# Splitting the wait of the score block and ordering its matmuls by head parity in a linear-attention and two-layer MoE kernel

## The chip, the cores and the metric

The kernel runs on one core of a Trainium2 chip. A core has five engines that run side by side, each through its own instructions in order: PE (TensorE, matrix multiplies), DVE (VectorE), ACT (ScalarE), POOL (GpSimd) and SP (SyncE, which here only issues DMA transfers). They order each other through semaphores. The metric is the device time of one execution in microseconds, lower is better.

## The reference, cut to what matters

Three layers follow each other: a recurrent attention over 768 steps for 4 x 8 (batch, head) pairs with a head dimension of 48, and two mixture-of-experts layers over the 3072 tokens. The change touches the first alone.

```python
B, H, S, D = r.shape                       # 4, 8, 768, 48
state = np.zeros((B, H, D, D))
for t in range(S):
    kt, vt, rt, wt = k[:, :, t], v[:, :, t], r[:, :, t], w[:, :, t]
    cur = np.einsum('bhd,bhe->bhde', u[None] * kt, vt)
    y[:, :, t] = np.einsum('bhd,bhde->bhe', rt, state + cur)
    state = wt[:, :, :, None] * state + np.einsum('bhd,bhe->bhde', kt, vt)
# then: top-1 MoE with softmax gate (8 experts, 384 -> 1024 -> 384),
# then: capacity-bound assignment by sorted logits and a second MoE of the same size
```

## The kernel before

**Tiling.** The attention works on 24 chunks of 128 time steps (`NT`): six chunks (`C`) for each of four batch elements, all eight heads together. Heads go in pairs: `PR = 4` pairs `a`, and in a pair head `g = 0` lies on partitions 0 to 63 and head `g = 1` on partitions 64 to 127 (48 dimensions padded to `HP = 64`). With cumulated decays a chunk becomes a masked product of keys and receptances (the scores), times values, plus the carried state.

**One chunk, over the engines.** DVE scans the decays (`scan_after`, `scan_before`), makes `k_dec` (`decay_k`, line 682, signals `s_kdec`), `rk`, and masks the scores (`mask_scores`, line 698). POOL makes `r_dec` (line 467, `s_rdec`). PE computes the scores in `score` (lines 814 to 825): for each pair and each `g` one float32 matmul of the 64 rows of `k_dec` and `r_dec` of that half, with 128 columns, into PSUM tile `p_g[0]` or `p_g[1]`. The last matmul of either tile signals `s_g`. DVE's `mask_scores(t)` waits for `s_g` twice, once for a tile, writes `scores` and signals `s_masked` twice. `values(t)` on PE multiplies the masked scores with the values.

**Order of the work.** The orders are written by hand, one loop over `t` for each engine. PE's loop in step `t` runs `score(t+1)`, `diag_sums(t+1)`, `update(t)` (state), `x_forward(t-1)`, `diag_back(t+1)`, `values(t)`, `logits(t-1)`, now and then `counts`, `k_transposes(t+1)` (in each sixth chunk `scored`, a product of expert weights with the gate, in its place) and `x_back(t)`. DVE's loop in step `t` runs `take_x(t-1)`, both scans of `t+2`, `mask_scores(t+1)`, `add_state(t)`, `decay_k(t+2)`, `product(t+2)` and parts of the routing. ACT moves results out of PSUM between PE's blocks: `diag_evac` (line 539) between `diag_sums` and `diag_back`, `k_evac`, `carry` of the state, `check` of the decays. SP loads decays, keys and receptances three chunks ahead, values one.

**What guards the tiles.** `score(t)` waits for `s_kdec` and `s_rdec` of `t`, and before it overwrites `p_g` for both masks of chunk `t - 1`: `s_masked >= 2 * t`. `decay_k(t + 1)` waits for both `s_g` of `t - 1`, since it overwrites a `k_dec` buffer. Behind the last chunk `first_h` uses the two `p_g` tiles for the first rows of the expert layer.

Of the kernel before, what the change touches and what calls it, by code (L numbers as in the profile page):

```python
# [19 lines left out]
PR = H // 2  # L20
HP = 64
# [174 lines left out]
def attention(nc, general, sb, ps, sem, io, keep):  # L196
# [78 lines left out]
    s_g = sem("s_g")  # L275
    s_masked = sem("s_masked")
# [54 lines left out]
    with nc.Block() as block:  # L331
# [481 lines left out]
        def _(pe):  # L813
            def score(t):
                pe.wait_ge(s_kdec, t + 1)
                pe.wait_ge(s_rdec, t + 1)
                if t > 0:
                    pe.wait_ge(s_masked, 2 * t)
                for a in range(PR):
                    for g in range(2):  # L820
                        half = slice(HP * g, HP * g + HP)
                        ins = pe.matmul(p_g[g][:, a, :], k_dec[half, t % 2, a, :], r_dec[half, t % 3, a, :],
                                        start=True, stop=True)
                        if a == PR - 1:
                            ins.then_inc(s_g, 1)

            def x_forward(t):
                pe.wait_ge(s_x, t + 1)
# [141 lines left out]
            for t in range(-1, NT):  # L970
                if t + 1 < NT:
                    score(t + 1)
                    diag_sums(t + 1)
# [8 lines left out]
                if t == 1:  # L982
                    pe.wait_ge(s_norm, 10)
                    for a in range(KD):
                        ins = pe.transpose(p_e[:, a, :], emb[:, a * P:(a + 1) * P], ident[0:E, 0:E])
# [1505 lines left out]
```

## Time and profile before

| | us |
|---|---|
| median of 3 runs | 824.91 |
| lowest, highest | 824.82, 826.84 |
| the profiled execution | 824.82 |
| its span in the profile | 823.0 |
| PE busy | 779.0 (95%) |
| DVE busy | 437.2 (53%) |
| ACT busy | 322.5 (39%) |
| attention stage, about | 0 to 188 |

The profile shows one execution. For each engine it has the busy time, and for each idle stretch the event that ended it. A float32 matmul leaves two records of PE and two of its weight loads (PEld, which run beside PE's matmuls), a transpose one. The end of a matmul record is modelled: records overlap, so the time from one start to the next tells what a matmul costs in a stream, not its duration.

### The profile page before, as it was taken

What the parts mean: (1) busy time and instruction counts of PE and PEld (TensorE: products, weight loads), DVE (VectorE), ACT (ScalarE), POOL (GpSimd) and SP (SyncE); (2) the same over time, 40 slices, a digit from 0 to 9 for tenths busy, and PEclk for the clock granted to TensorE, in tenths of its full rate; (3) what the DMA queues carried; (4) which work ended last, traced back from release to release, by engine and by line L of the source; (5) the groups of instructions that cost most, each with busy time, mean ns of one, the idle gap of its engine ahead of it and who ended that gap; (6) DMA issues with size and microseconds to landing.
All of it is one profiled execution on the core that took longest, in us unless ns stands there. A gap on an engine that the chain in (4) does not pass through costs nothing. (4 is left out here: it accounts for less than half of the span.)

```text
span 823.0 us, 17288 instructions
## 1 busy us (share of the span) xinstructions
PE 779.0 (95%) x6003; PEld 563.0 (68%) x6004; DVE 437.2 (53%) x1194; ACT 322.5 (39%) x818; POOL 145.0 (18%) x151
## 2 busy tenths in 40 slices
PE   8999999997999999999999965999999999999996
PEld 7778787865777778887777744755565555555653
DVE  8889898934333233333332348475767667573000
ACT  4878787843344444444444420112121211112120
POOL 4124343430000000000000000103223140502201
PEclk9999999999999999999999985999999999999999
DMA  8889899525677565667575511341505052346100
GB/s 278 312 274 355 310 348 326 216 82 188 219 251 250 198 208 201 208 227 268 179 262 191 169 52 63 121 154 58 192 20 192 33 189 94 124 151 218 49 10 31
DMA packets 68850, 149.63 MB, mean 182 GB/s; under 512 B 4968, under 2 KB 37104, under 8 KB 68784
## 3 DMA queue, kind: packets, MB, share of 16 engines
q1 hardware_dynamic: 53952, 114.03, 39.4%
q0 software_dynamic: 6912, 23.75, 8.5%
q10 hardware_dynamic: 7920, 10.99, 4.1%
q8 instruction: 39, 0.64, 0.3%
q14 instruction: 27, 0.22, 0.1%
HBM read 130.06 MB, written 18.69 MB: 181 GB/s over the span
## 5 line engine op out<-in xcount | busy, mean ns | idle before, releaser
L1498 PE MATMUL p_o<-w2s,hid_t 128*128 (+1 forms) x432 | 152.1, 495 | 0.0
L1487 PEld LDWEIGHTS p_h<-x_t,w1s 128*128 128x128 f32 x1248 | 143.4, 192 | 7.2
L1487 PE MATMUL p_h<-x_t,w1s 128*128 128x128 f32 x1248 | 143.5, 275 | 0.0
L1971 PE MATMUL p_gh<-g_t,w1s 128*128 128x384 f32 x384 | 132.8, 494 | 0.0
L1987 PE MATMUL p_go<-w2s,g_hid 128*128 128x384 f32 x384 | 131.5, 489 | 0.0
L1498 PEld LDWEIGHTS p_o<-w2s,hid_t 128*128 128x128 f32 x432 | 78.7, 192 | 45.9 <-issue 0.9
L1971 PEld LDWEIGHTS p_gh<-g_t,w1s 128*128 128x128 f32 x384 | 70.0, 190 | 45.7 <-issue 6.1
L1987 PEld LDWEIGHTS p_go<-w2s,g_hid 128*128 128x128 f32 x384 | 70.3, 190 | 42.1
L1371 ACT ACTIVATE hid_t<-p_h 128x512 f32<-128x512 f32 x52 | 31.0, 597 | 155.2 <-PE p_h L1487 144.8
L1710 ACT ACTIVATE g_hid<-p_gh 128x384 f32<-128x384 f32 x64 | 31.4, 490 | 112.8 <-PE p_gh L1971 112.8
L1671 POOL DMA_INDIRECT g_in<-y_rows,table x24 | 29.6, 1232 | 252.2 <-DVE table L1830 247.3
L1424 DVE TENSOR_SCALAR col<-col 128x1 f32<-128x1 f32 x27 | 4.2, 154 | 130.5 <-ACT ex L1375 130.4
L1760 DVE TENSOR_TENSOR reach<-free_best,cand 128x3968 bf16<-128x3968 f32 (+2 forms) x19 | 58.6, 3083 | 0.6
L1681 POOL DMA_INDIRECT out<-o_row,table x24 | 40.1, 1672 | 79.6 <-ACT o_row L1703 44.8
L518 ACT ACTIVATE diag_v<-v_pad,diag 128x48 f32<-128x48 f32 x192 | 48.0, 327 | 0.0
L467 POOL TENSOR_TENSOR r_dec<-kr_t,decays 128x512 f32<-128x512 f32 x24 | 28.7, 1197 | 103.7 <-issue 60.4
L1703 ACT ACTIVATE o_row<-p_go 128x384 f32<-128x384 f32 x24 | 11.8, 490 | 87.7 <-PE p_go L1987 87.7
L1696 ACT ACTIVATE g_t<-p_gx 128x384 f32<-128x384 f32 x22 | 10.8, 490 | 75.4 <-PE p_gx L1958 75.4
L1375 ACT ACT_TABLE_LOAD x27 | 34.6, 1283 | 3.7 <-issue 3.2
L1822 DVE TENSOR_TENSOR row_is<-row_b,iota_p 128x2048 bf16<-128x2048 bf16 (+1 forms) x16 | 34.9, 2221 | 0.3
L1358 ACT ACT_TABLE_LOAD x27 | 34.6, 1283 | 0.5
L1331 POOL COPY w2s<-w2g 128x64 f32<-128x64 f32 x6 | 1.4, 236 | 185.2 <-PE p_o L1498 185.2
(269 smaller groups left out, 1052.7 us busy)
## 6 DMA issues: line engine op xcount, KB each, us to landing
w1s<-in_w SPq DMA_DIRECT2D x28, 1536.0 KB, 6.6
kr_t<-in_kr_t SPq DMA_DIRECT2D x24, 512.0 KB, 4.0
w2t<-in_w_t SPq DMA_DIRECT2D x16, 768.0 KB
w1s<-in_w1b SPq DMA_DIRECT2D x8, 1536.0 KB, 6.6
w2s<-in_w2b SPq DMA_DIRECT2D x8, 1536.0 KB
w2s<-in_w POOLq DMA_DIRECT2D x12, 768.0 KB, 6.5
w_pad<-in_w_t SPq DMA_DIRECT2D x24, 256.0 KB, 5.0
v_pad<-in_v_pad SPq DMA_DIRECT2D x24, 256.0 KB, 7.9
```

The source lines that it names most:

```text
L518: ins = act.activation(diag_v[:, t % 2, h, :], v_pad[:, q, h, 0:D], ACT.Copy, scale=diag[:, t % 2, h:h + 1])
L1358: act.activation(col[:, q, 0:1], col[:, q, 15:16], ACT.Sqrt).then_inc(s_root, 1)
L1371: act.activation(hid_t[:, half * g:half * (g + 1), :], p_h[g][:, :, :], ACT.Relu).then_inc(s_relu, 1)
L1375: act.activation(ex[:, :], lg[:, q, :], ACT.Exp, bias=col[:, q, 9:10], accum_out=col[:, q, 10:11]).then_inc(s_exp, 1)
L1487: ins = pe.matmul(p_h[g][:, m, :], w1s[:, q, a, f:f + P], x_t[:, q, a, :], start=(a == 0), stop=(a == KD - 1))
L1498: ins = pe.matmul(p_o[:, :], hid_t[:, m, :], w2s[:, bass.ds(half, 1), m, :].rearrange("p o n -> p (o n)"), start=(m == 0), stop=(m == KF - 1))
L1681: pool.indirect_dma_start(out=io["out"][:, :], out_offset=place(1, p, i), in_=o_row[:, p % 2, i, :], in_offset=None).then_inc(s_out[p % 2] ...
L1710: act.activation(hid[:, m, :], p_h[(KF * p + m) % 3][:, :], ACT.Relu).then_inc(s_relu, 1)
L1760: dve.tensor_tensor(reach(n)[:, at, :], free(p)[:, at].unsqueeze(2).broadcast_to([P, len(part), n]), cand[:, 0:n].unsqueeze(1).broadcast_t ...
L1822: dve.tensor_tensor(row_is[:, at, :], row_b[:, 1, at].unsqueeze(2).broadcast_to([P, size, P]), iota_p[:, :].unsqueeze(1).broadcast_to([P, ...
L1971: ins = pe.matmul(p_h[n % 3][:, :], w1s[:, p % 2, a, m * P:(m + 1) * P], x_t[:, a, :], start=(a == 0), stop=(a == KD - 1))
L1987: ins = pe.matmul(p_o[n % 2][:, :], hid[:, m, i * P:(i + 1) * P], w2s[:, p % 2, m, 0:HD], start=(m == 0), stop=(m == KF - 1))
```

## The change

In `score` the two loops change places: first the four matmuls of `g = 0`, then the four of `g = 1`. The wait on `s_masked` is split: ahead of the `g = 0` matmuls for the first mask of chunk `t - 1`, ahead of the `g = 1` matmuls for the second. `s_g` is signalled by the fourth and by the eighth matmul, where it was the seventh and the eighth. The matmuls themselves, their operands and their number stay.

```diff
             def score(t):
                 pe.wait_ge(s_kdec, t + 1)
                 pe.wait_ge(s_rdec, t + 1)
-                if t > 0:
-                    pe.wait_ge(s_masked, 2 * t)
-                for a in range(PR):
-                    for g in range(2):
-                        half = slice(HP * g, HP * g + HP)
+                for g in range(2):
+                    half = slice(HP * g, HP * g + HP)
+                    if t > 0:
+                        pe.wait_ge(s_masked, 2 * (t - 1) + g + 1)
+                    for a in range(PR):
                         ins = pe.matmul(p_g[g][:, a, :], k_dec[half, t % 2, a, :], r_dec[half, t % 3, a, :],
                                         start=True, stop=True)
-                        if a == PR - 1:
-                            ins.then_inc(s_g, 1)
+                    ins.then_inc(s_g, 1)
```

What stands in PE's order at a score block of the running loop, before. The row's end names the semaphores that the first matmul waits for; the block begins behind `x_back` (line 927) and ends at `diag_sums` (line 856):

```order
L927 MATMUL p_x<-ident,y_tr 128x128 [waits s_xTev,s_yev]
L927 MATMUL p_x<-ident,y_tr 128x128 x3
L822 MATMUL p_g0<-r_dec,k_dec 128x128 [waits s_masked,s_rdec,s_kdec]
L822 MATMUL p_g1<-r_dec,k_dec 128x128
L822 MATMUL p_g0<-r_dec,k_dec 128x128
L822 MATMUL p_g1<-r_dec,k_dec 128x128
L822 MATMUL p_g0<-r_dec,k_dec 128x128
L822 MATMUL p_g1<-r_dec,k_dec 128x128
L822 MATMUL p_g0<-r_dec,k_dec 128x128
L822 MATMUL p_g1<-r_dec,k_dec 128x128
L856 MATMUL p_diag<-rk,u_blk 32x128 [waits s_diag,s_rk]
```

And with the change, at the same place (line numbers behind the function are one lower):

```order
L926 MATMUL p_x<-ident,y_tr 128x128 [waits s_xTev,s_yev]
L926 MATMUL p_x<-ident,y_tr 128x128 x3
L822 MATMUL p_g0<-r_dec,k_dec 128x128 [waits s_masked,s_rdec,s_kdec]
L822 MATMUL p_g0<-r_dec,k_dec 128x128 x3
L822 MATMUL p_g1<-r_dec,k_dec 128x128 [waits s_masked]
L822 MATMUL p_g1<-r_dec,k_dec 128x128 x3
L855 MATMUL p_diag<-rk,u_blk 32x128 [waits s_diag,s_rk]
L855 MATMUL p_diag<-rk,u_blk 32x128 x3
```

The tiles `p_g0` and `p_g1` alternated; now four of one stand ahead of four of the other, with a wait between.

The first score block of the kernel, behind the filler matmuls of line 122, which has no wait on masks, before:

```order
L122 MATMUL p_y<-ones 128x128 x19
L822 MATMUL p_g0<-r_dec,k_dec 128x128 [waits s_kdec,s_rdec,s_shape,s_in]
L822 MATMUL p_g1<-r_dec,k_dec 128x128
L822 MATMUL p_g0<-r_dec,k_dec 128x128
L822 MATMUL p_g1<-r_dec,k_dec 128x128
L822 MATMUL p_g0<-r_dec,k_dec 128x128
L822 MATMUL p_g1<-r_dec,k_dec 128x128
L822 MATMUL p_g0<-r_dec,k_dec 128x128
L822 MATMUL p_g1<-r_dec,k_dec 128x128
L856 MATMUL p_diag<-rk,u_blk 32x128 [waits s_rk]
```

and with the change:

```order
L122 MATMUL p_y<-ones 128x128 x19
L822 MATMUL p_g0<-r_dec,k_dec 128x128 [waits s_kdec,s_rdec,s_shape,s_in]
L822 MATMUL p_g0<-r_dec,k_dec 128x128 x3
L822 MATMUL p_g1<-r_dec,k_dec 128x128 x4
L855 MATMUL p_diag<-rk,u_blk 32x128 [waits s_rk]
L855 MATMUL p_diag<-rk,u_blk 32x128 x3
```

Here too only the order within the block moved.

## Rows read from the trace of the kernel before

**Rows 1.** The page: busy tenths in 40 slices, and the granted clock

```profile
PE   8999999997999999999999965999999999999996
...
DVE  8889898934333233333332348475767667573000
...
PEclk9999999999999999999999985999999999999999
```

**Rows 2.** Table by stretch: from:to, length, busy of each engine; six chunks each

```profile
49.00:90.20 41.20, 40.54 (x551) 31.83 (x550) 37.69 (x75) 32.75 (x114) 14.46 (x11) 1.00 0.91 328
...
131.50:172.80 41.30, 40.59 (x551) 31.85 (x550) 34.16 (x71) 32.74 (x114) 14.85 (x12) 1.00 0.62 216
```

**Rows 3.** Timeline of PE, one chunk: start, length, line, tiles, count

```profile
108.17 0.63 PE L919 MATMUL p_kb<-ident,k_dec 128*128 128x128 f32 x4
108.64 0.60 PE L927 MATMUL p_x<-ident,y_tr 128*128 128x128 f32 x4
109.17 1.16 PE L822 MATMUL p_g<-r_dec,k_dec 64*128 64x128 f32 x16
110.27 0.43 PE L856 MATMUL p_diag<-rk,u_blk 128*32 128x128 f32 x8
...
116.02 1.16 PE L822 MATMUL p_g<-r_dec,k_dec 64*128 64x128 f32 x16
```

**Rows 4.** Waits of PE's weight loads, 8 to 176: total, times, longest

```profile
PEld p_diag L862 <- ACT diag_t L539: 4.4, 10, 1.8
PEld p_u L889 <- issue: 4.0, 20, 0.2
PEld p_y L847 <- issue: 3.9, 23, 0.2
...
PEld p_g L822 <- DVE k_dec L682: 2.9, 6, 0.8
```

**Rows 5.** Waits of PE's matmuls in the same stretch

```profile
PE p_g L822 <- DVE k_dec L682: 1.7, 3, 0.6
PE p_diag L862 <- ACT diag_t L539: 1.6, 1, 1.6
PE p_x L830 <- DVE rows L717: 0.3, 1, 0.3
```

**Rows 6.** Waits of DVE in the same stretch

```profile
DVE rows L717 <- PE p_x L927: 8.2, 4, 4.1
...
DVE scores L698 <- PE p_g L822: 0.3, 1, 0.3
```

**Rows 7.** Timeline of DVE over the same chunk

```profile
110.05 0.56 DVE L717 TENSOR_TENSOR rows<-p_x,diag_v 128x384 f32<-128x384 f32 x1
...
113.31 1.26 DVE L698 TENSOR_TENSOR scores<-p_g,mask 128x512 f32<-128x512 f32 x2
...
114.75 0.68 DVE L682 TENSOR_TENSOR k_dec<-kr_t,decays 128x512 f32<-128x512 f32 x1
```

**Rows 8.** Timeline of PE, one score block in growing cuts

```profile
102.79 0.38 PE L822 MATMUL p_g<-r_dec,k_dec 64*128 64x128 f32 x2 [0.59 <-DVE k_dec L682]
102.79 0.60 PE L822 MATMUL p_g<-r_dec,k_dec 64*128 64x128 f32 x6 [0.59 <-DVE k_dec L682]
102.79 1.16 PE L822 MATMUL p_g<-r_dec,k_dec 64*128 64x128 f32 x16 [0.59 <-DVE k_dec L682]
```

**Rows 9.** The score line's matmul (least, median, most), then full-height ones

```profile
L822 PE MATMUL p_g<-r_dec,k_dec x384: 272/272/373, 8.8 to 164.6; 64*128 64x128 f32 x192
...
184.03 2.75 PEld L965 LDWEIGHTS p_g<-x_t,w1s 128*128 128x128 f32 x24
184.05 2.92 PE L965 MATMUL p_g<-x_t,w1s 128*128 128x128 f32 x24
```

**Rows 10.** Timeline at the end of the stage

```profile
176.98 0.64 PE L927 MATMUL p_x<-ident,y_tr 128*128 128x128 f32 x4
...
187.00 0.96 POOL L478 DMA_INDIRECT sorted_rows<-rows,pos  x1 [2.47 <-DVE pos L770]
```

## What I expect of the change, and why

> **What bounds the kernel now.** I read the slices first, to place the edited function. It runs only in the attention stage, the first ten of the 40 slices, where PE and DVE both show eights and nines at full clock [rows 1]; everything behind it (the expert layers, the assignment) is untouched. The table by stretch then splits the stage into runs of six chunks (one batch element each): 41.2 to 41.3 us each, PE busy for 40.5 to 40.6 of them, DVE for 34 to 38 (two of the runs stand in [rows 2]). Two engines this full need to be told apart by who waits for whom. In PE's order of time for one chunk the blocks stand back to back: the score block starts at 109.17, diag_sums at 110.27 (its last record modelled to end at 110.33), and so on to the next score block at 116.02 [rows 3]. In 168 us PE's weight loads wait for other engines for only some 8 us [rows 4], and PE itself waits for k_dec 1.7 us in all [rows 5]. DVE waits for PE 8.2 us, in four places, one behind each long w2·w_gate block [rows 6]. So PE sets the pace, DVE is close behind, and nearly every nanosecond added to PE's stream shows in the end.
>
> **The change, part by part.** It does three things to the 24 score blocks: it splits the wait on s_masked, it moves the first s_g signal, and it changes the order of the eight matmuls from g0, g1, g0, g1... to four of g0 and then four of g1.
>
> *The wait.* It could give something only if score(t) waited for the masks of chunk t-1. It can't: DVE makes k_dec(t) behind both masks of t-1 in its own order (113.31, then 114.75) [rows 7], and the block waits for k_dec(t) as well. s_masked has always been reached when s_kdec is. Gain: 0. The added wait inside the block is met for the same reason. Its cost I take from the nearest pair of blocks with a met wait between them and no change of tile shape, k_transposes to x_back: four matmuls start at 108.17 and the next block at 108.64, 0.117 us per matmul, no gap [rows 3]. So 0; the upper bound is the 0.17 to 0.20 us of idle that PE's loads show as "issue" ahead of blocks, 20 to 23 times a line [rows 4]. Behind this wait stand the g1 matmuls and all that PE does later, but it is never the last to come.
>
> *The signal.* mask_scores(t) starts some 4 us after its score block (109.17 against 113.31) [rows 3, 7], and in the whole stage DVE waited for p_g once, 0.3 us [rows 6]. An earlier p_g0 is worth 0. A p_g1 that is 0.8 us later still leaves 2 us of cover; if the masks moved up against the block, that cover would be gone and the delay would be DVE's too.
>
> *The order.* This is the term that counts. The block is 16 matmul records (each of the 8 float32 matmuls leaves two) of 64 rows by 128 columns. Cut into short stretches, the records come in pairs: two give 0.38 us, six 0.60, sixteen 1.16, so a pair takes 0.11 us ((1.16 - 0.38) / 7 = 0.111) [rows 8]. Full-height matmuls of the same 128 columns, which can't share the array, take that long for a single record: 24 records in 2.92 us give (2.92 - 0.27) / 23 = 0.115 (0.27 is one matmul from start to end, the least in the group of the score line) [rows 9]. So the two halves of the array work side by side now, since neighbours in PE's order use different halves (rows 0 to 63 for g0, 64 to 127 for g1). After the change neighbours use the same half. Eight records of g0 at 0.111 each, the last of them beside the first of g1, then seven more of g1: the block grows by 7 x 0.111 = 0.78 us, to 1.94. Bounds: 6 x 0.111 = 0.67 if one more record slips beside another, 8 x 0.111 = 0.89 if g1 starts only behind g0.
>
> The Trainium skill has two rules on this, in "TensorE: Matmul & The Clock Gate", Part 3, The mechanism: matmuls start strictly in program order, which makes the 0.78; and a weight load overlaps a running matmul only where its row group differs. The second would make it worse, and is the third rival below.
>
> *What of it is hidden.* Chunk 0: diag_back(0) waited 1.6 us for ACT's diag_t behind score(0) [rows 5], so all of its 0.78 goes. The other 23 give 23 x 0.78 = 17.9 us of PE time. Against that stand PE's waits for others, which a slower PE fills: k_dec in three blocks, 1.7 us [rows 5]; take_x once, 0.3 [rows 5]; diag_t, 4.4 us over 10 times by the loads, less the 1.8 of chunk 0, 2.6 over nine, of which some 0.1 each is the step between blocks that stays, so 1.7 [rows 4]. In sum 3.7. They can be filled because the waited-for engines get a longer period too: ACT's diag_t hangs on k_evac and check behind PE's k_transposes, and the score block lies between these and diag_back. Late next, when PE is slower: nobody. DVE's 8.2 us of waiting only grows.
>
> The stage so ends 17.9 - 3.7 = 14.2 us later. Its last link is PE's too (x_back(23) at 176.98, on which take_x, the logits and the last scatter at 187.00 hang) [rows 10], so what follows starts later by the same amount, and its own work is unchanged. The profiled execution took 824.82 (span 823.0) and is 0.09 under the median of 824.91, so both bases give 839.0 to 839.1. **Forecast: 839.0 us, slower by 1.7%.**
>
> **The rivals.**
>
> *The order doesn't matter to the array (not slower).* The matmul queue holds g1's work while g0's runs; if each half of the array took its own next matmul as soon as it was free, the block would stay at 1.16 us and the time at 824.9. Place: the 24 score blocks. It decides below 23 x d - 3.7 = 2.5, that is for d under 0.27 us a block. For it: the pairs of today start practically together. Against it: that shows two neighbours in program order together, never one that overtakes; nothing in the trace does.
>
> *DVE takes over as the bound.* DVE is busy for 37.7 of 41.2 us [rows 2] and has no visible gap in the chunk shown. If its order of work held the next block back by a fixed time, PE's growth would be swallowed in half of the chunks: 824.8 + (17.9 - 3.7) / 2 = 832. Against: from take_x at 110.05 to k_dec's end at 115.43 are 5.4 us [rows 7], while PE's period becomes 6.4 to 6.9 plus 0.78.
>
> *Loads no longer hidden.* In the first pair of a block the load is exposed: 0.38 us for two records against 0.27 for one shows some 0.1 us. If loads into the same half waited for its matmul each time, records would come 0.21 us apart: 15 x 0.21 + 0.27 = 3.4 us a block, 23 x 2.26 - 3.7 = 48, time 873. Against: the full-height matmuls of [rows 9], which all share every row of the array, load 128 columns each and still come 0.115 apart, with loads of 2.75 us beside matmuls of 2.92. This is the skill's second rule; the row speaks against it as it stands.
>
> *More than the sum.* g1 starts behind g0 (0.89 us) and nothing is filled: 23 x 0.89 = 20.5, time 845.3.
>
> **How the numbers follow.** Forecast 0.74 (its own range from 835.2, with 0.67 us a block and 5 us filled, to 842, with 0.78 and 1 us filled); more than the sum 0.09; DVE the bound 0.07; the order doesn't matter 0.06; loads exposed 0.04. The range must leave out no more than 2 in 10: from 834.0, just above the half-swallowed case, to 845.5, the case in which nothing is filled. What a measurement can tell here is about 0.3%, 2.5 us: slower 0.93, within 0.06, faster 0.01, since no part of the change shortens a path.
>
> **What the profile after should show.** The group of score matmuls keeps its 384 records, but a block goes from 1.16 to about 1.94 us, short stretches growing by one record per 0.11 us. A run of six chunks goes from 41.3 to about 45 (six times 0.78 less about 1.1 filled). PE's waits for k_dec and for diag_t go to nearly nothing, DVE's for PE (take_x) spread over all chunks, the masks still wait for nothing, and all behind the attention stage is the same length. A block of 1.2 us would prove the first rival, one of 3 us the third; a block of 1.9 with a run of six under 43 would prove DVE the bound.

## The result, and the profile after

The change makes the kernel slower: 832.65 us median (831.70 to 835.03, six runs) beside 825.88 for the kernel before (824.69 to 828.62, six runs). The ratio is 1.0094, with a 95% interval of 1.0078 to 1.0111, so +7.8 us, between +6.4 and +9.2 (the two medians lie 6.8 us apart, inside that interval). The prediction had the sign and the place right, but forecast 839.0 us, with a range that began at 834.0.

The page of the change, the rows that answer to [rows 1]: tenths of busy time in 40 slices, and the granted clock.

```profile
PE   8999999997999999999999983999999999999996
...
DVE  7889898955333333233233327666857686673000
...
PEclk9999999999999999999999995899999999999998
```

PE's first ten slices are as full as before; nothing in them shows the loss. The table by stretch does. Two runs of six chunks, from score block to score block, in the columns of [rows 2]:

```profile
52.90:96.15 43.25, 43.25 (x552) 35.02 (x551) 38.01 (x75) 33.02 (x114) 14.47 (x11) 1.00 0.88 315
96.15:139.40 43.25, 43.25 (x552) 35.05 (x551) 38.09 (x75) 33.03 (x114) 15.51 (x13) 1.00 0.92 319
```

A run of six takes 43.25 us where it took 41.2 to 41.3, and PE is busy in all of it (43.25 of 43.25, where 0.7 us were idle). DVE's share falls to 38 of 43. One score block in growing cuts (timeline of PE), as [rows 8] shows it of before:

```profile
115.97 0.71 PE L822 MATMUL p_g<-r_dec,k_dec 64*128 64x128 f32 x4
...
115.97 0.93 PE L822 MATMUL p_g<-r_dec,k_dec 64*128 64x128 f32 x6
...
115.97 1.71 PE L822 MATMUL p_g<-r_dec,k_dec 64*128 64x128 f32 x16
```

The block lasts 1.71 us, 0.55 more than before (1.16), not 0.78 more. The cuts say why. The first ends 0.53 us behind the block's start, and four records have begun; the second ends 0.56 us behind it, and six have. In between, g0's fifth record has started (at 0.55 us) and a second one beside it. That one is g1's first: it has the long duration of a half's first record (373 ns, the most in [rows 9]), and g0's sixth to eighth stand ahead of it in PE's order. Who waits for whom has turned as forecast. The waits of PE's loads for other engines and of DVE for PE, 8 to 184 us (total, times, longest), as [rows 4] and [rows 6]:

```profile
PEld p_g L822 <- issue: 3.7, 22, 0.2
...
PEld p_diag L861 <- ACT diag_t L539: 1.6, 1, 1.6
```

```profile
DVE rows L717 <- PE p_x L926: 10.9, 7, 5.4
...
DVE scores L698 <- PE p_g L822: 1.9, 2, 1.3
```

The one wait for diag_t that is left is that of chunk 0. Those of the running loop, 2.6 us in nine places, are gone, and the 2.9 us for k_dec with them. DVE's take_x (`rows`, line 717) waits in seven places instead of four.

**The length of the stage in one number.** x_back is the last block of each chunk on PE, so the time from its first to its last start spans chunks 0 to 23 and holds the score blocks of chunks 2 to 23, 22 of them. The line's own row says both (first and last start). Before, and with the change:

```profile
L927 PE MATMUL p_x<-ident,y_tr x96: 272/273/329, 18.7 to 177.3; 128*128 128x128 f32 x96
```

```profile
L926 PE MATMUL p_x<-ident,y_tr x96: 272/273/329, 21.8 to 187.1; 128*128 128x128 f32 x96
```

158.6 us before, 165.3 us with the change: +6.7. The score block of chunk 1 stands ahead of it; with its +0.55 that is +7.3 us, which agrees with the 7.8 of the ratio.

**What not to read from the two first profiles.** Their spans differ by 4.5 us only (823.0 and 827.5), less than the stage alone. In the profile of the change x_back also starts 3.1 us later (21.8 beside 18.7), in part because the granted clock was at its lower level for some of the first 18 us, which experiments 2 and 4 take up. What hides most of both is the search in the second expert layer's assignment; first the kernel before, then the same kernel in another execution (experiment 4), first and last start of its matmuls:

```profile
L1925 PE MATMUL p_search<-takers,reach x713: 166/166/190, 493.2 to 724.8; 128*128 128x8 bf16 x117, 128*31 128x8 bf16 x62
```

```profile
L1925 PE MATMUL p_search<-takers,reach x713: 165/167/190, 492.9 to 720.8; 128*128 128x8 bf16 x117, 128*31 128x8 bf16 x62
```

231.6 us in the one, 227.9 in the other, for the same program. With the change it is 227.9 too (501.8 to 729.7). The experiments were run in four series: 1 to 4, 5 to 8, 9 to 12 and 13 to 16. They agree within themselves, not with each other. The kernel before measured 822.0 us in the first, 826.4 in the second, 822.7 in the third and 827.0 in the fourth, and the search of every kernel took 227.9 to 228.0 us in the first and third and 231.5 to 232.3 in the others. Each series ran on another chip (numbers 15, 0, 9 and 4 on record), so the chip is the nearest suspect; chip and time of the run were not told apart. So a stretch is compared between profiles only where the same kernel repeats it (the 158.6 us stand in four profiles of before or of its order: before, experiments 2, 4 and 13), and times only within a series.

### The profile page after: what moved, and what is told of

Its sections match the earlier page's. It is cut to its first block and busy times, and to the rows that moved or that the text cites. A ratio compares the mean times of both kernels' runs of the same rounds, so it can differ in the third digit from the quotient of the medians.

```text
span 827.5 us, 17288 instructions
## 1 busy us (share of the span) xinstructions
PE 790.9 (96%) x6003; PEld 577.1 (70%) x6004; DVE 438.1 (53%) x1194; ACT 323.3 (39%) x818; POOL 148.7 (18%) x151
## 5 line engine op out<-in xcount | busy, mean ns | idle before, releaser
L1680 POOL DMA_INDIRECT out<-o_row,table x24 | 43.8, 1825 | 79.7 <-ACT o_row L1702 44.8
L822 PE MATMUL p_g<-r_dec,k_dec 64*128 64x128 f32 x384 | 41.0, 285 | 1.3 <-DMA u_blk<-in_u_blk 1.3
L822 PEld LDWEIGHTS p_g<-r_dec,k_dec 64*128 64x128 f32 x384 | 36.4, 187 | 5.2 <-issue 3.7
L663 DVE TENSOR_TENSOR_SCAN decays<-w_pad,last 128x520 f32<-128x520 f32 x24 | 29.9, 1244 | 11.6 <-ACT state L575 9.3
## 6 DMA issues: line engine op xcount, KB each, us to landing
w2s<-in_w2b SPq DMA_DIRECT2D x8, 1536.0 KB, 10.1
```

The source lines that it names most:

```text
L1680: pool.indirect_dma_start(out=io["out"][:, :], out_offset=place(1, p, i), in_=o_row[:, p % 2, i, :], in_offset=None).then_inc(s_out[p % 2] ...
```

## The experiments

All are edits of the kernel before unless said. "Stage" is the time from the first to the last start of x_back. A ratio is that of a kernel's time to the time of the kernel before in the same series, with its 95% interval. The diffs are shortened to the lines that matter.

**1. The order alone.** One wait on both masks ahead of the block, then four g0, four g1.

```diff
                 if t > 0:
                     pe.wait_ge(s_masked, 2 * t)
-                for a in range(PR):
-                    for g in range(2):
+                for g in (0, 0, 0, 0, 1, 1, 1, 1):   # a counts up in each g
```

> The order of the change with the single wait on both masks ahead of the block, as before. In the profile of the change a block has its first g1 matmul beside the fifth of the eight g0 records (0.556 us behind the block's start, g0's fifth at 0.550), and lasts 1.71 us from first start to last end against 1.16. Theory A (the order alone does it: the half-array of g1 can start at most about three records ahead of its turn): block 1.71 us, time as with the change, 1.009 of before. Theory B (the wait in the middle holds g1 back or lets it go at that point; without it g1 may run freely ahead): the block is shorter, down to 1.2 us, and the time within 1.003 of before.

Ratio 1.0081 (1.0061 to 1.0102), stage 165.3 us, and the block is the change's to the hundredth:

```profile
114.44 1.71 PE L823 MATMUL p_g<-r_dec,k_dec 64*128 64x128 f32 x16
```

So the wait in the middle neither holds g1 back nor lets it go: the order alone makes the loss. Theory A stands.

**2. The wait alone.** Order g0, g1, g0, g1, the second mask's wait ahead of the first g1 matmul.

```diff
-                if t > 0:
-                    pe.wait_ge(s_masked, 2 * t)
                 for a in range(PR):
                     for g in range(2):
+                        if t > 0 and a == 0:
+                            pe.wait_ge(s_masked, 2 * (t - 1) + g + 1)
```

> The order of before (g0, g1, g0, g1...), with the wait split: the first mask ahead of the first g0 matmul, the second mask ahead of the first g1 matmul. Theory A: the wait is always met and costs nothing, block 1.16 us, ratio 1.000 with an interval that holds 1. Theory B: the wait in the block costs some 0.1 to 0.2 us a block, of which 2 to 5 us in all less what other waits of PE fill; ratio up to 1.002.

Ratio 1.0014 (1.0001 to 1.0028), block 1.16 us, stage 158.6 us: the stage is the one of before. By the ratio alone the question stays open, since its interval just leaves out 1; block and stage decide for theory A. What its profile has beside the stage is a start that is 2 us longer, taken up under experiments 13 to 16.

**3. Runs of two.**

```diff
-                for a in range(PR):
-                    for g in range(2):
+                for g in (0, 0, 1, 1, 0, 0, 1, 1):
```

> Single wait ahead, order g0 g0 g1 g1 g0 g0 g1 g1: runs of four records for each half. Theory A (a record can start while up to three ahead of it in program order have not started): g1's first record starts with g0's first, and from there all pairs run side by side, so the block stays at 1.16 us and the ratio at 1.000. Strict program order (which the prediction used): only the neighbours at the three borders overlap, 13 steps of 0.111 us instead of 8, block 1.7 us, ratio about 1.009.

Ratio 1.0009 (0.9995 to 1.0022), stage 159.0 us. The block is 1.26 us, not 1.16 and far from 1.7:

```profile
109.94 1.26 PE L823 MATMUL p_g<-r_dec,k_dec 64*128 64x128 f32 x16
```

So program order is not kept between the halves, which is where the prediction's sum failed. The 0.10 us over 1.16 were not expected. By the starts of its records they are one step of 0.21 us instead of 0.11, behind the first record of g1's second run; behind the first record of any block there is such a step too. Behind the first record of g0's second run there is none, so it isn't simply the price of a new run, and its cause is open.

**4. The kernel before again.**

> The kernel before, unchanged, for a second profile of it. It tells which differences between the two first profiles belong to the execution and not to the change: score(0) waiting 1.3 us for u_blk against 0.3, the clock of 0.72 between 12 and 18 us against 1.00, and the stretch from 520 to 750 us, 3.9 us shorter in the profile of the change. If they are noise, ratio 1.000, and at least one of them differs from the first profile of before. If they belonged to the change, this profile repeats the first one in all three.

Ratio 1.000 (0.9987 to 1.0013), span 817.6 us, stage 158.6. One of the three differences is shown here to be none of the change's: the search took 227.9 us, as in the profile of the change. The other two repeat the first profile: the wait for u_blk is short (0.4 us), and the clock between 12 and 18 us is 1.00. That both can differ without the change's order is seen in experiment 2, where the wait is 0.8 us and the clock 0.72.

**5, 6. More PE time without another order.** The first pair of matmuls is issued twice (experiment 5) or four times (experiment 6).

```diff
-                for a in range(PR):
+                for a in [0] * 3 + list(range(PR)):      # [0] * 1 in experiment 5
                     for g in range(2):
```

> The kernel before with the first pair of matmuls (a = 0, g0 and g1) issued twice in each score block, in the alternating order: two record pairs more, 0.22 us more PE time, same results. Theory A (only PE's time counts, and PE's own waits of some 5 us are filled first): 23 x 0.22 = 5.1 us, of which about 4 fill waits for k_dec, diag_t and take_x; ratio 1.001. Rival (nothing is filled): 1.006.

> As the last, with the first pair issued four times: 0.67 us more in each block, without any change of the order. Theory A: 23 x 0.67 - 5.0 = 10.4 us, ratio 1.0126, and the change, whose block grew by 0.55 us in its profile, lies on the same line (23 x 0.55 - 5.0 = 7.6, 1.009). Rival (the order or the late s_g of g1 costs something beside PE's time): this kernel is no slower than the change, though its blocks are longer.

Experiment 5: 1.0012 (1.0001 to 1.0023), stage 160.2 us. Experiment 6: 1.0085 (1.0068 to 1.0102), stage 168.2:

```profile
L927 PE MATMUL p_x<-ident,y_tr x96: 272/273/331, 19.6 to 187.8; 128*128 128x128 f32 x96
```

The stages follow PE's time: 22 x 0.22 = 4.9 us make it 1.6 longer, 22 x 0.67 = 14.7 make it 9.6 longer, and the change lies between them with 22 x 0.55 = 12.1 and 6.7. What is missing was filled into waits: 3.3, 5.1 and 5.4 us. Above some 0.5 us a block there is hardly more to fill. So the order costs what it adds to PE's time, and no more: the rival, by which experiment 6 would be no slower than the change, has the stage against it (9.6 beside 6.7 us), and in one series of runs too, with filler in both, 834.4 beside 832.5 us (experiments 16 and 14). But the ratio of experiment 6 is too low for its stage: 9.6 and 0.7 for chunk 1 are 10.3 us, 1.0125, and 1.0125 is outside the interval. That was left to experiments 10 and 13 to 16.

**7. Runs of three.**

```diff
-                for a in range(PR):
-                    for g in range(2):
+                for g in (0, 0, 0, 1, 1, 1, 0, 1):
```

> Order g0 g0 g0 g1 g1 g1 g0 g1, one wait ahead: runs of six records. Theory A (a record can start while at most three ahead of it have not started): g1's first record starts beside g0's third, two steps late, and the first load of g1 is exposed for 0.1 us as in the change; block 1.16 + 0.22 + 0.1 = 1.48 us, 23 x 0.32 - about 4.5 = 3 us, ratio 1.0036. If instead half of each run overlaps whatever its length, g1 starts three steps late: block 1.6 us, ratio 1.006.

Ratio 1.0031 (1.0017 to 1.0046), stage 161.2 us, block as theory A has it:

```profile
111.81 1.49 PE L823 MATMUL p_g<-r_dec,k_dec 64*128 64x128 f32 x16
```

**8. diag_back behind values.**

```diff
-                if t + 1 < NT:
-                    diag_back(t + 1)
...
                 if 0 <= t < NT:
                     values(t)
+                if t + 1 < NT:
+                    diag_back(t + 1)
```

> The kernel before with diag_back(t + 1) moved behind values(t) on PE, so that the transposes no longer wait for ACT's diag_t; the score block is as before. Theory A (PE sets the pace, its waits are time of the stage): the ten waits of 0.18 to 0.28 us for diag_t go, 2.2 us, some of which may come back as waits for k_dec; ratio 0.997 to 0.9985. Rival (ACT and DVE are as much the bound): diag_out comes later, diag_v and with it take_x too, and the ratio is 1.000 or above.

Ratio 0.9946 (0.9927 to 0.9966): better than theory A had it, faster than both kernels. The stage is 155.1 us, 3.5 shorter:

```profile
L927 PE MATMUL p_x<-ident,y_tr x96: 272/273/331, 19.0 to 174.1; 128*128 128x128 f32 x96
```

```profile
PEld p_g L822 <- DVE k_dec L682: 4.4, 9, 1.0
```

The waits for diag_t are gone (2.6 us), and the k_dec waits grew from 2.9 to 4.4 us: part came back, as the theory said. The other 2.4 us are not in these waits, but in PE's steps: with the transposes of diag_back right ahead of it, logits hands over to the next block 0.59 us behind its start, where it took 0.69 (from 114.10 to 114.79 us before, from 112.00 to 112.59 here), and so in each of 22 chunks, 2.2 us in all. Why logits is shorter in that place was not tried apart.

**9. Runs of eight.** Each half gets its first matmul five times, eight g0 and then eight g1.

```diff
-                for a in range(PR):
-                    for g in range(2):
+                for g in range(2):
+                    for a in [0] * PR + list(range(PR)):
```

> Each half gets its first matmul (a = 0) five times, so that eight g0 matmuls stand ahead of eight g1 matmuls: runs of 16 records, one wait ahead, results unchanged. Theory A (at most three records not yet started may be passed, whatever the length of the run): g1's first record starts beside g0's 13th of 16, 1.44 us behind the block's start, and the block lasts 3.5 us. Rival (g1 joins at the middle of the run, as it did beside the fifth of eight in the change): g1 starts beside the ninth, at 1.0 us, and the block lasts 3.05 us.

```profile
103.37 1.60 PE L822 MATMUL p_g<-r_dec,k_dec 64*128 64x128 f32 x12
...
103.37 1.82 PE L822 MATMUL p_g<-r_dec,k_dec 64*128 64x128 f32 x14
...
103.37 3.50 PE L822 MATMUL p_g<-r_dec,k_dec 64*128 64x128 f32 x32
```

The first cut ends 1.43 us behind the block's start, and twelve records have begun; the second at 1.47, and two more have: g0's 13th and g1's first. The block lasts 3.50 us. It is three records that are passed, not half of a run. The kernel took 870.15 us in its one run.

**10. Experiment 6 again.**

> The same kernel as the one with the first pair issued four times, which measured 1.0085 (interval 1.0068 to 1.0102) though its profile has the attention stage 10 us longer. If the low ratio was that chip's scatter (start of the kernel, other executions of before), this one gives 1.010 to 1.014. If a stage behind the attention gives time back when the attention is this late, it repeats 1.0085, and its profile has a stretch behind the attention shorter than in the profiles of before.

Ratio 1.0081 (1.006 to 1.0103), stage 167.8. The low ratio repeats, so the first expectation fails. The second fails too: no stretch behind the attention is shorter than in experiment 4. From the last start of x_back to the first of the search it is 315.1 us here and 315.0 there, and the search is 227.9 us in both. What stands out is the spread: its six runs lie within 0.8 us (828.84 to 829.60), those of before in the same series within 4.8 (819.88 to 824.71). The fastest of each are 9.0 us apart, the medians 6.6.

**11. The change and diag_back behind values.** The edits of the change and of experiment 8 together.

> The change together with diag_back behind values. Theory A (PE's stream sets the time, and a wait can be filled only once): diag_later alone took 3.5 us off the stage; with the change on top only k_dec's waits are left to fill, about 3 us, so the stage is 22 x 0.55 - 3 = 9 us longer than with diag_later alone, some 5.5 us longer than before with the score block of chunk 1; ratio 1.0065 to 1.008. Rival (the effects simply add): 1.0085 - 0.0054 = 1.003 to 1.004.

Ratio 1.0056 (1.0032 to 1.008), stage 164.2 us, 9.1 longer than with experiment 8 alone, as computed. The interval holds theory A's 1.0065 and the rival's 1.004, so the time alone doesn't decide; the stage does, for A. As in experiment 6 the ratio is lower than the stage has it (5.6 us and 0.55 for chunk 1 would be 1.0075). A wait that is gone cannot be filled: the change costs 9.1 us in the stage here, 6.7 without the better order.

**12. rk on POOL.** Experiment 8, with the product k * r moved from DVE to POOL ahead of decay_r.

```diff
+            def product(t):                       # now in POOL's program, pool. for dve.
...
                 if t + 2 < NT:
+                    product(t + 2)
                     decay_r(t + 2)
```

> The order of before, diag_back behind values, and the product rk (0.69 us a chunk) moved from DVE to POOL, ahead of its decay_r. In the profile of diag_later PE's loads still waited 4.4 us for DVE's k_dec, in nine places, of which some 3 us are more than the step between blocks. Theory A (with diag_t gone DVE's k_dec is the last to come, and DVE is relieved by 0.6 us a chunk): those 3 us go, ratio 0.991 to 0.993. Rival (POOL's rk, at POOL's 1.2 us for a product of this size, comes later than DVE's or slows DVE beside it): diag_sums waits for it, ratio 0.995 or above.

Ratio 1.0118 (1.0093 to 1.0142). The rival had named the cause, a POOL that slows DVE beside it, but had diag_sums wait for it and not the score block, and no more of a figure than "0.995 or above". Groups of instructions (behind the count: busy us, mean ns of one), experiment 12 and then before:

```profile
L672 DVE TENSOR_TENSOR_SCAN decays<-w_pad,last 128x520 f32<-128x520 f32 x17 | 27.6, 1622 | 1.7 <-ACT state L584 1.6
...
L475 POOL TENSOR_TENSOR rk<-kr_t 128x512 f32<-128x512 f32 x17 | 22.9, 1345 | 0.4
...
L741 DVE SCALAR_TENSOR_TENSOR c_at_best<-c_at_best,rank_of 128x24 f32<-128x24 f32 x7 | 9.9, 1420 | 0.2
...
L771 DVE CAST pos<-pos_f 128x3 uint32<-128x3 f32 x6 | 7.5, 1255 | 0.2
```

```profile
L663 DVE TENSOR_TENSOR_SCAN decays<-w_pad,last 128x520 f32<-128x520 f32 x17 | 21.0, 1236 | 3.0 <-ACT state L575 2.8
...
L740 DVE SCALAR_TENSOR_TENSOR c_at_best<-c_at_best,rank_of 128x24 f32<-128x24 f32 x6 | 1.1, 184 | 0.2
...
L770 DVE CAST pos<-pos_f 128x3 uint32<-128x3 f32 x6 | 1.0, 170 | 0.2
```

The means mix instructions beside POOL's product with others. One by one, some DVE operations that run beside it grow by 1.0 to 1.7 us, where the product itself takes 1.3: the 24-element operation takes 1906 to 1927 ns in five places and 183 to 185 in two, the scan 2232 to 2896 in six places and 1219 to 1243 in 16. Others don't. Least, median and most of DVE's `rows`, which reads the PSUM tile p_x and ran beside the product five times:

```profile
L718 DVE TENSOR_TENSOR rows<-p_x,diag_v x22: 539/548/559, 23.1 to 174.9; 128x384 f32<-128x384 f32 x22
```

And POOL's other product of this size, r_dec, has always run beside the masks, 46 of 48 of them before, and they read PSUM too; all 48 took 664 to 692 ns. So what POOL's product costs depends on the operation that DVE runs meanwhile. Here it turned the relief into a wait: k_dec came later, and PE's loads waited 12.7 us for it. A second loss came with these waits. Twice, behind a PE that had waited 1.4 us for k_dec, the granted clock fell to the lower level for some 3 us in the middle of the stage:

```profile
109.00:112.00 3.00, 3.00 (x38) 2.39 (x38) 2.98 (x2) 1.62 (x5) 1.90 (x2) 0.50 1.06 313
```

The stage is 168.8 us, 13.7 longer than in experiment 8.

**13 to 16. Filler at the start.** In four kernels, 23 instead of 20 filler matmuls ahead of score(0), and six behind diag_sums(0): before (13), the change (14), experiment 8 (15), experiment 6 (16).

```diff
-            keep_busy(pe, 20, p_y[:, 0, :], ones)
+            keep_busy(pe, 23, p_y[:, 0, :], ones)
...
                     diag_sums(t + 1)
+                if t == -1:
+                    keep_busy(pe, 6, p_y[:, 0, :], ones)
```

> The kernel before with filler matmuls where PE idles at the start: 23 instead of 20 ahead of the first score block, and six more behind diag_sums(0). The second profile with the order of before (wait split) and the profile of the change had the granted clock at 0.72 between 12 and 18 us and reached score(1) 2 us later than the others. Theory A (the idle time ahead of it costs the clock in some executions): with the filler none is late, the runs lie closer together, median 0.5 to 1.5 us lower, ratio 0.998 to 0.9995. Rival (the clock falls there whatever PE does, or the filler delays the first blocks): ratio 1.000 or above.

> The change with the same filler at the start. Theory A: the stage's growth is unchanged, so 1.0088 less what the filler gives, 1.0070 to 1.008. Rival (what the change lost beyond its stage came from the start): nearer to 1.006.

> Order of before, diag_back behind values, and the filler. Theory A: the gain of diag_later (0.9946, its stage 3.5 us shorter) and that of the filler add: ratio 0.993 to 0.995. Rival: the first ratio was partly scatter, 0.996.

> The first pair issued four times, with the filler. Without it this kernel measured 1.0085 and 1.0081, where its stage in both profiles is 10 us longer (1.0125), and its runs lay within 1.4 us while those of before spread over 5. Theory A (its longer score(0) already kept the clock up, so that it never paid what before pays in some executions): the filler gives it nothing, ratio again 1.008 to 1.0085, and its distance to the kernel before with filler grows towards 1.010. Rival (a gain behind the attention): the distance to before with filler stays 1.008.

| experiment | median us | ratio to before (95%) | to experiment 13 | stage us |
|---|---|---|---|---|
| 13, before and filler | 824.29 | 0.9974 (0.9962 to 0.9986) | | 158.6 |
| 14, change and filler | 832.47 | 1.0068 (1.0049 to 1.0087) | +8.2 | 165.7 |
| 15, experiment 8 and filler | 820.30 | 0.992 (0.9902 to 0.9938) | -4.0 | 155.1 |
| 16, experiment 6 and filler | 834.43 | 1.0093 (1.0075 to 1.0111) | +10.1 | 168.2 |

Filler makes the kernel before 2.7 us faster by the medians, where 0.5 to 1.5 were expected; ten of its twelve runs lie within 1.3 us. The ratio of experiment 14 falls between its two expectations, that of experiment 15 just under its own. Measured from there, experiment 6 costs 10.1 us (experiment 16), where its stage and chunk 1 say 10.3. Experiment 14 costs 8.2, where 7.1 and 0.55 stand in its stage and chunk 1. So the 3 us that experiment 6 lacked are a matter of the kernel it was compared with: with filler in both they are there. What the kernel before pays in some executions, and experiment 6 doesn't, is only partly seen. One piece stands at the start. The row of 12 to 18 us (PE's busy time first, the granted clock third from the end), and the filler of line 122, in experiments 4 and 2, which have the same order of PE's work:

```profile
12.00:18.00 6.00, 5.56 (x74) 4.93 (x76) 5.93 (x9) 3.38 (x12) 2.30 (x4) 1.00 0.96 313
...
13.04 2.17 PE L122 MATMUL p_y<-ones 128*128 128x128 f32 x18
```

```profile
12.00:18.00 6.00, 5.32 (x39) 5.04 (x39) 4.96 (x7) 2.45 (x7) 2.30 (x4) 0.72 0.96 304
...
13.28 3.73 PE L122 MATMUL p_y<-ones 128*128 128x128 f32 x18
```

The same 18 records take 2.17 us at full clock and 3.73 where the clock fell to its lower level for part of them, behind a PE that had waited 1.9 us for diag_t. In experiment 4 PE had waited as long, 1.9 us, and the clock stayed, so the wait alone doesn't decide. In experiment 13 filler stands in that wait:

```profile
10.52 1.60 PE L122 MATMUL p_y<-ones 128*128 128x128 f32 x12
...
12.44 0.33 PE L862 MATMUL p_diag<-ident,diag_t 128*128 128x128 f32 x1 [0.32 <-ACT diag_t L539]
...
13.05 2.17 PE L122 MATMUL p_y<-ones 128*128 128x128 f32 x18
```

PE waits 0.3 us, and the clock stays. But this can't be all of it. Of the 14 profiles without filler only two have the fall at the start (the change and experiment 2), too few to move a median by 2.7 us, and x_back starts no earlier with filler (19.3 us in experiment 13, as in experiment 4). A larger piece stands in the pause behind the attention. Experiments 3 and 4, of one series, have spans of 823.6 and 817.6 us with nearly the same stage; the rows of 188 to 218 us:

```profile
188.00:218.00 30.00, 23.08 (x102) 16.07 (x103) 11.33 (x51) 9.46 (x19) 0.00 (x0) 0.83 0.50 177
```

```profile
188.00:218.00 30.00, 26.04 (x141) 19.64 (x142) 12.10 (x55) 12.06 (x23) 0.00 (x0) 0.94 0.56 193
```

PE idles 3.0 us longer there in experiment 3 and has the lower clock for longer, and the search starts 5.8 us later. Which of the two pieces the filler takes away, and by what, isn't shown. Against the kernel before of its series, experiment 15 is the fastest of the study, by 0.8%.

## Why the prediction was wrong, point by point

*What bounds the kernel.* Right. PE set the pace: the stage followed PE's time in every kernel (1.6, 6.7 and 9.6 us for 0.22, 0.55 and 0.67 us a block), and DVE, named as the close second, only waited more for PE.

*The wait and the signal: 0.* Right. Experiment 2's stage is that of before. The masks waited for p_g in two places instead of one, 1.9 us in all, with 1.3 as the longest, against the forecast that they would still wait for nothing. The stage doesn't show it: the change stays on the line of experiments 5 and 6, which left the signals on the last two matmuls.

*The order, 0.78 us a block.* The step that failed: 0.55 us were measured. That records of one half come one by one, 0.11 us apart, was right. That the halves overlap only where neighbours meet, as strict program order would have it ("matmuls start strictly in program order"), was not. The first rival had them free of the order. The runs show something between: a record may start ahead of up to three of the other half. In runs of two, three, four and eight matmuls g1's first record started beside g0's first, third, fifth and thirteenth. The lower bound of 0.67 us, "if one more record slips beside another", was set one record from the forecast, though nothing in the trace of before could tell one from four: there, neighbours always used different halves. The bound ought to have reached to the rival's 0.

*What is hidden, 3.7 us.* Mis-sized too: 5.4 us were filled. Two of the terms were taken too low, k_dec from the loads' 2.9 us [rows 4] to the matmuls' 1.7 [rows 5], diag_t from 2.6 to 1.7, for a step between blocks that I took as staying. The loads' own waits, 2.9 + 2.6 + 0.5 for take_x = 6.0, would have been the nearer bound. The sum with both terms as measured: 23 x 0.55 - 5.4 = 7.3 us, against 7.8 measured. (The 5.4 are what the stage leaves over, so this compares the stage with the time and is no separate check of the term.) The order is the larger error: 0.55 in place of 0.78 takes 5.3 us off the forecast, 5.4 in place of 3.7 only 1.7.

*The rivals.* Rival one (the order doesn't matter) was a third of the truth: it took 0.23 of the 0.78 us off. DVE as the bound, and loads that are not hidden, fell: the records of a half stay 0.11 us apart, each with its own load beside the matmul ahead of it, in the run of sixteen too. So the Trainium skill's rule on weight loads ("TensorE: Matmul & The Clock Gate", Part 3, The mechanism), as the third rival took it, doesn't hold here for two loads into the same half, and its rule that matmuls start in program order does not hold between the halves: g1's first record starts while three of g0 that precede it have not. Within a half nothing here speaks against it.

*The range.* Its lower end, 834.0, was put between the forecast's own lower bound (835.2) and the case of DVE as the bound (832), with the first rival at 824.9 left outside. A mixture of forecast and rival was not among the cases, and that is where the time fell.

## What to carry to other kernels

Matmuls that use one half of the array each should alternate in PE's order, or come in runs of two at the most. With runs of two, three and four matmuls (four, six and eight records) a block of sixteen records was 0.10, 0.33 and 0.55 us longer here. Where an in-order engine sets the pace, its visible waits are what an added piece may use up before it costs, and what a better order can win: moving one short block behind a long one gave 0.5%. The two don't add: a wait that a better order removes can no longer hide an added piece (the change cost the stage 6.7 us alone, 9.1 on top of experiment 8). When two mechanisms are rivals, their mixture is a case too, and the range must span it.

## What the runs showed of the hardware

- PE starts a matmul record of one half of the array ahead of up to three records of the other half that stand before it in its program, and no more in any block of these runs (float32, 64 rows, 128 columns; experiments 1, 3, 7 and 9).
- The step behind a half's first record in a block is 0.21 us instead of 0.11. With runs of two there is one more such step, in g1's second run (block 1.26 us); with runs of three there is none in the second runs (1.49 us = 1.16 + 0.33). The cause is open.
- Beside POOL's 128x512 float32 product (1.3 us) a DVE operation of 24 elements takes 1.9 us instead of 0.18 and a scan 2.2 to 2.9 instead of 1.24 (experiment 12). DVE operations that read PSUM kept their time beside it (0.54 us) and beside POOL's other product of this size (0.66 to 0.69 us).
- The granted clock fell to its lower level behind a PE that had waited 1.3 to 1.9 us (the change and experiment 2 between 12 and 18 us, twice in experiment 12), and not behind each such wait (experiment 4).
- The same program's search takes 227.9 us in some series of runs and 231.6 in others, each series on another chip. The cause is open.
